# First expert layer of a mixture of experts: 16 products of 128 tokens in place of 8 of 256, per block of hidden units

## The chip, the cores and the metric

The kernel runs on one core of one Trainium2 chip. The metric is the device time of one execution in microseconds; the kernel before has a median of 1494.01 us over two runs (1491.9 and 1496.12).

## What is computed

Three stages follow one another: a recurrent attention, a mixture of eight experts with two experts per token, and a dense two-layer network. The change touches the second, which the reference writes so (N = 3072 tokens, D = 320, E = 8 experts, F = 1024 hidden units):

```python
for e in range(E):
    for k in range(2):
        mask = top2[:, k] == e
        if not mask.any():
            continue
        h = np.maximum(x[mask] @ w1[e], 0.0)
        out[mask] += top2_w[mask, k, None] * (h @ w2[e])
```

## The kernel before

The function `stage_re` first routes: it sorts the (token, expert) pairs by expert into tiles of TS = 256 rows, 31 tiles in all (NTS), each belonging to one expert. The routing ends with small products at line 1000 that turn positions into source rows. Then the function `tile` runs once per tile on every engine; tiles 0, 1 and the last are written out, the others run in a loop of two.

All products of a tile are done in the type float32r, and each operand is split into a high part and a low remainder, so that a product of two operands is three matmuls: high by high, high by low and low by high. ScalarE writes the high parts (`split_hi`, line 814), VectorE the remainders (`split_lo`, line 819).

On TensorE a tile has three parts:

- First layer (lines 963 to 974). For each of NF = 8 blocks `f` of 128 hidden units, the 320 inputs are taken in slices j = 0, 1 (three matmuls each, lines 970 to 972) and a last slice of 64 inputs, whose high and low rows are stacked to 128 (two matmuls, lines 973 and 974). The stationary operand, which is loaded ahead of each matmul, is a 128 x 128 block of the expert's weights (`w1h`, `w1l`); the moving operand is the tile's 256 tokens (`xh`, `xl`). The eight matmuls of a block add up in one PSUM bank (banks 2 to 5 in turn), and the last one raises the semaphore `e_mm1`.
- The turn of the next tile's rows (`turn`, line 954): six transposes against the identity.
- Second layer (lines 985 to 987). For each block `f` and each half `s` of 128 tokens, three matmuls with the tokens' activations as the stationary operand and 320 columns of `w2h` or `w2l` as the moving one.

ScalarE waits for `e_mm1` of a block before it makes `hh` (line 1029), VectorE then makes the remainder `hl` (line 1104), which the second layer needs, and which frees the PSUM bank for block f + 4. POOL gathers the rows of the tile after next once the transposes of a tile are done (line 1072). SP issues the weight loads.

Each of the 31 tiles thus has 8 x 8 = 64 first-layer matmuls: 1984 in all. In the attention stage the products of line 615 (`rows`) are of plain float32, in which one matmul of the code shows as two records in the trace, each with its own load of weights; those of line 1000 are of float32r, with one record each.

Of the kernel before, what the change touches and what calls it, by code (L numbers as in the profile page):

```python
# [821 lines left out]
def stage_re(nc, st, w_in, w_out, w1, w2, xrow, ysort):  # L822
    ctx = ExitStack()
    with ctx:
        def sb(name, shape, dt=F32):
            return ctx.enter_context(nc.sbuf_tensor(name, shape, dt))

        def sem(name):
            return ctx.enter_context(nc.semaphore(name))
# [5 lines left out]
        NF, NS = F1 // 128, TS // 128  # L835
# [5 lines left out]
        w1h, w1l = (sb(n, [128, 3, F1], F32R) for n in ("w1h", "w1l"))  # L841
        w2h, w2l = (sb(n, [128, NF, DM], F32R) for n in ("w2h", "w2l"))
        xs = sb("xs", [128, 2, NS, DM])
        xh = sb("xh", [128, 3, TS], F32R)
        xl = sb("xl", [128, 2, TS], F32R)
# [48 lines left out]
        q = {n: sem(n) for n in names}  # L894
# [5 lines left out]
        def tiles(eng, tile):  # L900
            tile(0, 0, 0, True, False)
            tile(1, 1, 0, True, False)
            with eng.Fori(1, NTS // 2) as n:
                tile(n * 2, 0, n, False, False)
                tile(n * 2 + 1, 1, n, False, False)
            tile(NTS - 1, 0, NTS // 2, False, True)
# [38 lines left out]
        @block.tensor  # L945
        def _(pe):
            mm = nc.tensor.matmul

            def turn(i, p, n):
                pe.wait_ge(gx[p], n * GX + GX)  # L950
                for j, (k0, kr) in enumerate(KE):
                    for s in range(NS):
                        c0 = (j % 2) * TS + s * 128
                        m = nc.tensor.transpose(ps[j // 2][0:kr, c0:c0 + 128], xs[:, p, s, k0:k0 + kr], ident[:, :])  # L954
                m.then_inc(q["e_tr"], 1)

            def tile(i, p, n, first, final):
                if first and p == 0:
                    turn(0, 0, 0)
                pe.wait_ge(q["e_xl"], i * 2 + 2)  # L960
                pe.wait_ge(q["e_w1l"], i * 3 + 3)
                for f in range(NF):
                    fs = slice(f * 128, f * 128 + 128)
                    o = ps[2 + f % 4][:, 0:TS]
                    if f >= 4:
                        pe.wait_ge(q["e_hl"], i * NF + (f - 3))
                    elif not (first and p == 0):
                        pe.wait_ge(q["e_hl"], i * NF - (3 - f))
                    for j in range(2):
                        mm(o, w1h[:, j, fs], xh[:, j, :], start=(j == 0), stop=False)  # L970
                        mm(o, w1h[:, j, fs], xl[:, j, :], start=False, stop=False)  # L971
                        mm(o, w1l[:, j, fs], xh[:, j, :], start=False, stop=False)  # L972
                    mm(o, w1h[:, 2, fs], xh[:, 2, :], start=False, stop=False)
                    mm(o, w1l[:, 2, fs], xh[:, 2, :], start=False, stop=True).then_inc(q["e_mm1"], 1)  # L974
                if not final:
                    turn(i + 1, 1 - p, n + p)
                if not (first and p == 0):
                    pe.wait_ge(q["e_yA"], i)
                    pe.wait_ge(q["e_yV"], i)
                for f in range(NF):  # L980
                    pe.wait_ge(q["e_hl"], i * NF + f + 1)
                    pe.wait_ge(q["e_w2l"], i * NF + f + 1)
                    for s in range(NS):
                        o, sl = ps[6 + s][:, 0:DM], slice(s * 128, s * 128 + 128)
                        mm(o, hh[:, f, sl], w2h[:, f, :], start=(f == 0), stop=False)  # L985
                        mm(o, hh[:, f, sl], w2l[:, f, :], start=False, stop=False)  # L986
                        m = mm(o, hl[:, f, sl], w2h[:, f, :], start=False, stop=(f == NF - 1))  # L987
                m.then_inc(q["e_mm2"], 1)

            pe.wait_ge(q["r_M"], 1)  # L990
            mf = M.rearrange("p e i -> p (e i)")
            mm(ps[5][:, 0:E * NT], one[:, 0:128], mf, start=True, stop=True).then_inc(q["r_PR"], 1)
            mm(ps[4][:, 0:E * NT], triu[:, :], mf, start=True, stop=True).then_inc(q["r_PR"], 1)
            for z, h in enumerate((slice(0, NH0), slice(NH0, NHI))):
                pe.wait_ge(q["r_hi"], z + 1)
                for j in range(2):
                    for i in range(NT):
                        if z == 0 and i % 12 == 0:
                            pe.wait_ge(q["r_lo"], 2 * j + i // 12 + 1)
                        m = mm(ps[3 + 3 * z][:, h], lows[:, j, i, :], highs[:, j, i, h], start=(j + i == 0), stop=(j * i == NT - 1))  # L1000
                m.then_inc(q["r_Q"], 1)
            tiles(pe, tile)

        @block.scalar
# [486 lines left out]
```

## Time and profile before

| what | value |
| --- | --- |
| median of two runs | 1494.01 us |
| profiled execution | 1499.73 us |
| its span, first to last instruction | 1497.9 us |
| TensorE matmul busy | 1297.3 us, 87% of the span |
| weight loads busy | 1180.8 us, 79% |
| VectorE, ScalarE, POOL busy | 925.8, 656.7, 300.8 us |
| mean granted TensorE clock | 0.909 of full speed |

The profiled execution is 5.7 us (0.4%) above the median of the two timed runs, and 1.8 us of it lie outside the span. The stages follow each other: attention to about 560 us, routing to about 623 us, the expert tiles to about 1101 us, the dense network to the end. In the profile PE is TensorE's matmuls and PEld its weight loads, which run beside the matmuls. Where one matmul follows another, the records overlap, because each holds its own latency: how fast the engine goes is read from the distance between starts, not from the duration of one record.

### The profile page before, as it was taken

What the parts mean: (1) busy time and instruction counts of PE and PEld (TensorE: products, weight loads), DVE (VectorE), ACT (ScalarE), POOL (GpSimd) and SP (SyncE); (2) the same over time, 40 slices, a digit from 0 to 9 for tenths busy, and PEclk for the clock granted to TensorE, in tenths of its full rate; (3) what the DMA queues carried; (4) which work ended last, traced back from release to release, by engine and by line L of the source; (5) the groups of instructions that cost most, each with busy time, mean ns of one, the idle gap of its engine ahead of it and who ended that gap; (6) DMA issues with size and microseconds to landing.
All of it is one profiled execution on the core that took longest, in us unless ns stands there. A gap on an engine that the chain in (4) does not pass through costs nothing. (4 is left out here: it accounts for less than half of the span.)

```text
span 1497.9 us, 40886 instructions
## 1 busy us (share of the span) xinstructions
PE 1297.3 (87%) x16814; PEld 1180.8 (79%) x16814; DVE 925.8 (62%) x1605; ACT 656.7 (44%) x1453; POOL 300.8 (20%) x252
## 2 busy tenths in 40 slices
PE   3449877886989783999999999999949999999998
PEld 3337666675867662999999999999947888888887
DVE  5868578484745404678788787888734445454433
ACT  2314443342534231367677676767623332333332
POOL 3406243162612221211111111111023021020000
PEclk9966888787888995699999999999978999999999
DMA  6743453637232311487777878688712011010000
GB/s 164 194 94 122 124 172 109 153 108 191 95 82 92 104 50 48 136 269 225 259 232 237 258 225 263 211 253 245 226 53 71 18 36 44 10 53 18 0 18 18
DMA packets 158556, 197.77 MB, mean 132 GB/s; under 512 B 62581, under 2 KB 117085, under 8 KB 158429
## 3 DMA queue, kind: packets, MB, share of 16 engines
q1 hardware_dynamic: 134428, 149.66, 33.8%
q10 hardware_dynamic: 18721, 28.20, 6.2%
q0 software_dynamic: 5280, 18.03, 4.2%
q8 instruction: 103, 1.69, 0.5%
q14 instruction: 24, 0.20, 0.0%
HBM read 171.53 MB, written 24.31 MB: 131 GB/s over the span
## 5 line engine op out<-in xcount | busy, mean ns | idle before, releaser
L354 DVE TENSOR_TENSOR prod<-Tl,Lt 128x1 f32<-128x1 f32 (+30 forms) x186 | 147.9, 795 | 80.0 <-DMA Lt<-lscr 74.0
L1279 DVE TENSOR_TENSOR gf<-psM,low 128x512 f32<-128x512 f32 x96 | 66.4, 692 | 182.1 <-ACT low L1317 173.7
L1317 ACT ACTIVATE low<-psM 128x512 f32<-128x512 f32 x96 | 57.6, 600 | 245.3 <-PE psM L1375 218.6
L985 PE MATMUL psE<-w2h,hh 128*128 128x320 f32 x496 | 155.7, 314 | 0.0
L987 PE MATMUL psE<-w2h,hl 128*128 128x320 f32 x496 | 153.3, 309 | 0.0
L986 PE MATMUL psE<-w2l,hh 128*128 128x320 f32 x496 | 153.2, 309 | 0.0
L1072 POOL DMA_INDIRECT xs<-xrow,src x62 | 61.0, 984 | 408.9 <-PE psE L954 370.3
L970 PE MATMUL psE<-xh,w1h 128*128 128x256 f32 x496 | 141.0, 284 | 1.9 <-DVE xh L819 1.9
L971 PE MATMUL psE<-xl,w1h 128*128 128x256 f32 x496 | 140.9, 284 | 0.0
L972 PE MATMUL psE<-xh,w1l 128*128 128x256 f32 x496 | 140.9, 284 | 0.0
L819 DVE TENSOR_TENSOR w2l<-w2t,w2h 128x320 fp32r<-128x320 f32 x248 | 122.1, 492 | 16.8 <-ACT w2h L814 16.8
L1354 PE MATMUL psM<-woh,gh 128*128 128x320 f32 x384 | 120.3, 313 | 5.2 <-DVE gl L819 5.0
L1104 DVE SCALAR_TENSOR_TENSOR hl<-psE,hh 128x256 fp32r<-128x256 f32 x248 | 105.2, 424 | 22.6
L1356 PE MATMUL psM<-woh,gl 128*128 128x320 f32 x384 | 118.6, 309 | 0.0
L1355 PE MATMUL psM<-wol,gh 128*128 128x320 f32 x384 | 118.5, 309 | 0.0
L814 ACT ACTIVATE w2h<-w2t 128x320 fp32r<-128x320 f32 x248 | 115.0, 464 | 5.7 <-DMA w2t<-in_w_dram 5.1
L1029 ACT ACTIVATE hh<-psE 128x256 fp32r<-128x256 f32 x248 | 95.4, 385 | 47.2 <-PE psE L974 46.0
L819 DVE TENSOR_TENSOR w1l<-w1t,w1h 128x1024 fp32r<-128x1024 f32 (+1 forms) x93 | 108.1, 1218 | 2.0
L814 ACT ACTIVATE w1h<-w1t 128x1024 fp32r<-128x1024 f32 x93 | 91.4, 1050 | 13.9 <-DMA w1t<-in_w_dram 13.9
L970 PEld LDWEIGHTS psE<-xh,w1h 128*128 128x128 f32 x496 | 95.6, 193 | 2.3 <-DVE xh L819 2.3
L358 DVE TENSOR_REDUCE Tl<-prod 128x1 f32<-128x1 f32 (+30 forms) x186 | 93.7, 504 | 5.9
L972 PEld LDWEIGHTS psE<-xh,w1l 128*128 128x128 f32 x496 | 95.8, 193 | 0.0
(182 smaller groups left out, 3140.0 us busy)
## 6 DMA issues: line engine op xcount, KB each, us to landing
w2t<-in_w_dram SPq DMA_DIRECT2D x31, 1280.0 KB, 6.8
w1t<-in_w_dram SPq DMA_DIRECT2D x31, 1024.0 KB, 8.7
w1t<-in_w_dram SPq DMA_DIRECT2D x62, 256.0 KB, 9.3
Vd<-in_vG_dram ACTq DMA_DIRECT2D x44, 320.0 KB, 5.0
ysort<-ys SPq DMA_DIRECT2D x31, 320.0 KB, 4.9
RV<-in_rvE_dram ACTq DMA_DIRECT2D x44, 208.0 KB
P<-in_wR_dram SPq DMA_DIRECT2D x24, 209.6 KB
U<-in_wE_dram SPq DMA_DIRECT2D x24, 209.6 KB
```

The costliest lines, as they stand in the source:

```text
L354: mark(nc.vector.tensor_tensor(prod[:, 0:t, 0:t], Tl[:, 0:t, CH - t:CH], Lt[:, t:t + 1, CH - t:CH].to_broadcast([128, t, t]), ALU.mult))
L814: return nc.scalar.activation(hi, src, ACT.Copy)
L819: return nc.vector.tensor_tensor(lo, src, hi.bitcast(F32), ALU.subtract)
L970: mm(o, w1h[:, j, fs], xh[:, j, :], start=(j == 0), stop=False)
L971: mm(o, w1h[:, j, fs], xl[:, j, :], start=False, stop=False)
L972: mm(o, w1l[:, j, fs], xh[:, j, :], start=False, stop=False)
L985: mm(o, hh[:, f, sl], w2h[:, f, :], start=(f == 0), stop=False)
L986: mm(o, hh[:, f, sl], w2l[:, f, :], start=False, stop=False)
L987: m = mm(o, hl[:, f, sl], w2h[:, f, :], start=False, stop=(f == NF - 1))
L1354: mm(o, gh[:, f % 4, sl], woh[:, f, :], start=(f == 0), stop=False)
L1355: mm(o, gh[:, f % 4, sl], wol[:, f, :], start=False, stop=False)
L1356: m = mm(o, gl[:, f % 4, sl], woh[:, f, :], start=False, stop=(f == NF - 1))
```

## The change

The eight matmuls of a block are issued twice, first for tokens 0 to 127 and then for tokens 128 to 255 (NS = 2), each with 128 moving columns and into its own half of the same PSUM bank. Every matmul of the second half loads the weights anew that its partner in the first half had loaded. The semaphore is raised once, by the sixteenth matmul.

```diff
-                    for j in range(2):
-                        mm(o, w1h[:, j, fs], xh[:, j, :], start=(j == 0), stop=False)
-                        mm(o, w1h[:, j, fs], xl[:, j, :], start=False, stop=False)
-                        mm(o, w1l[:, j, fs], xh[:, j, :], start=False, stop=False)
-                    mm(o, w1h[:, 2, fs], xh[:, 2, :], start=False, stop=False)
-                    mm(o, w1l[:, 2, fs], xh[:, 2, :], start=False, stop=True).then_inc(q["e_mm1"], 1)
+                    for z in range(NS):
+                        zs = slice(z * 128, z * 128 + 128)
+                        oz = o[:, zs]
+                        for j in range(2):
+                            mm(oz, w1h[:, j, fs], xh[:, j, zs], start=(j == 0), stop=False)
+                            mm(oz, w1h[:, j, fs], xl[:, j, zs], start=False, stop=False)
+                            mm(oz, w1l[:, j, fs], xh[:, j, zs], start=False, stop=False)
+                        mm(oz, w1h[:, 2, fs], xh[:, 2, zs], start=False, stop=False)
+                        m = mm(oz, w1l[:, 2, fs], xh[:, 2, zs], start=False, stop=True)
+                    m.then_inc(q["e_mm1"], 1)
```

On TensorE, at the start of a tile inside the loop, the block that goes to bank 2 (psE2) and the first matmul of the next block (psE3) stand so before the change; behind the names are the columns of the weights and of the moving operand:

```order
L970 MATMUL psE2<-xh,w1h 128x256 [waits e_hl,e_w1l,e_xl]
L971 MATMUL psE2<-xl,w1h 128x256
L972 MATMUL psE2<-xh,w1l 128x256
L970 MATMUL psE2<-xh,w1h 128x256
L971 MATMUL psE2<-xl,w1h 128x256
L972 MATMUL psE2<-xh,w1l 128x256
L973 MATMUL psE2<-xh,w1h 128x256
L974 MATMUL psE2<-xh,w1l 128x256
L970 MATMUL psE3<-xh,w1h 128x256 [waits e_hl]
```

The last rows of the same block in the changed program, on the same engine, from the second half's first matmul on (lines 973 to 977 are the old 970 to 974):

```order
L973 MATMUL psE2<-xh,w1h 128x128
L974 MATMUL psE2<-xl,w1h 128x128
L975 MATMUL psE2<-xh,w1l 128x128
L973 MATMUL psE2<-xh,w1h 128x128
L974 MATMUL psE2<-xl,w1h 128x128
L975 MATMUL psE2<-xh,w1l 128x128
L976 MATMUL psE2<-xh,w1h 128x128
L977 MATMUL psE2<-xh,w1l 128x128
L973 MATMUL psE3<-xh,w1h 128x128 [waits e_hl]
```

The eight rows of one block have become sixteen, of half the moving columns and with the same waits ahead of the first; nothing else on TensorE, and nothing on any other engine, has moved.

## Rows read from the trace of the kernel before

**Rows 1.** Page: busy time of TensorE; its clock in 40 slices.
```profile
PE 1297.3 (87%) x16814; PEld 1180.8 (79%) x16814; DVE 925.8 (62%) x1605; ACT 656.7 (44%) x1453; POOL 300.8 (20%) x252
PEclk9966888787888995699999999999978999999999
```
**Rows 2.** Windows: length, then busy PE, PEld, DVE, ACT, POOL; clock, DMA share, GB/s.
```profile
600.00:1100.00 500.00, 497.74 (x3744) 497.16 (x3745) 393.59 (x738) 326.29 (x714) 61.03 (x62) 0.97 0.73 228
```
**Rows 3.** Groups by line: busy us, mean ns of one, idle before (us).
```profile
L970 PE MATMUL psE<-xh,w1h 128*128 128x256 f32 x496 | 141.0, 284 | 1.9 <-DVE xh L819 1.9
L971 PE MATMUL psE<-xl,w1h 128*128 128x256 f32 x496 | 140.9, 284 | 0.0
L972 PE MATMUL psE<-xh,w1l 128*128 128x256 f32 x496 | 140.9, 284 | 0.0
L973 PE MATMUL psE<-xh,w1h 128*128 128x256 f32 x248 | 70.3, 284 | 0.0
L974 PE MATMUL psE<-xh,w1l 128*128 128x256 f32 x248 | 70.3, 283 | 0.0
```
**Rows 4.** Timeline of PE over one tile: start us, us, then the instruction.
```profile
855.93 0.28 PE L970 MATMUL psE<-xh,w1h 128*128 128x256 f32 x1
...
863.61 0.82 PE L954 MATMUL psE<-ident,xs 128*128 128x128 f32 x6
864.18 0.39 PE L985 MATMUL psE<-w2h,hh 128*128 128x320 f32 x1
...
871.30 0.28 PE L970 MATMUL psE<-xh,w1h 128*128 128x256 f32 x1
```
**Rows 5.** Timeline of the weight loads of line 1000.
```profile
599.37 10.32 PEld L1000 LDWEIGHTS psE<-woh,wih 128*128 128x128 f32 x48 [9.74 <-issue]
610.17 10.31 PEld L1000 LDWEIGHTS psE<-woh,wih 128*128 128x128 f32 x48 [0.49 <-DVE woh L1180]
```
**Rows 6.** Groups by line, line 1000 and the loads of the first layer.
```profile
L1000 PE MATMUL psE<-woh,wih 128*128 128x56 f32 x48 | 10.4, 394 | 0.4 <-DVE woh L1180 0.4
L1000 PE MATMUL psE<-woh,wih 128*128 128x6 f32 x48 | 10.4, 353 | 9.3 <-DVE wih L1186 9.3
...
L1000 PEld LDWEIGHTS psE<-woh,wih 128*128 128x128 f32 x96 | 20.6, 332 | 10.2 <-issue 9.7 <-DVE woh L1180 0.5
...
L972 PEld LDWEIGHTS psE<-xh,w1l 128*128 128x128 f32 x496 | 95.8, 193 | 0.0
```
**Rows 7.** Timeline: the products of line 615, at full and at half clock.
```profile
211.40 1.86 PEld L615 LDWEIGHTS psA<-wx,xT 104*128 104x128 f32 x16 [0.19 <-issue]
211.40 2.02 PE L615 MATMUL psA<-wx,xT 104*128 104x96 f32 x16
...
566.96 3.49 PEld L615 LDWEIGHTS psA<-wx,xT 104*128 104x128 f32 x16 [0.95 <-DVE xT L378]
```
**Rows 8.** Windows: the granted clock is the third number from the right.
```profile
599.40:620.40 21.00, 20.60 (x96) 20.51 (x96) 14.66 (x11) 3.13 (x4) 5.05 (x4) 0.50 0.29 66
623.83:627.04 3.21, 3.21 (x15) 3.21 (x16) 0.00 (x0) 0.00 (x0) 0.62 (x1) 0.50 1.07 397
627.04:1101.00 473.96, 473.96 (x3638) 473.96 (x3638) 378.20 (x724) 322.30 (x708) 54.08 (x56) 1.00 0.75 234
128.00:132.00 4.00, 3.34 (x157) 2.89 (x156) 2.29 (x6) 1.35 (x4) 3.78 (x3) 1.00 0.02 4
132.00:136.00 4.00, 3.57 (x135) 2.61 (x138) 3.90 (x4) 1.03 (x1) 4.00 (x2) 0.51 0.26 67
```
**Rows 9.** Waits: engine, line, releaser: us in total, times, longest us.
```profile
POOL xs L1072 <- PE psE L954: 364.3, 28, 13.2
...
ACT hh L1029 <- PE psE L974: 46.0, 214, 0.2
```
**Rows 10.** Timeline of PE in the first tile.
```profile
623.83 0.58 PE L970 MATMUL psE<-xh,w1h 128*128 128x256 f32 x1 [1.86 <-DVE xh L819]
...
633.01 0.82 PE L954 MATMUL psE<-ident,xs 128*128 128x128 f32 x6
```

## The prediction

> **What bounds the kernel now.** I began with the page: TensorE's matmuls fill 87% of the span, more than any other engine's work, and its clock is high through the middle [rows 1]. The windows by stage say where that counts: in the 500 us of the expert tiles the matmuls are busy 497.7 us, VectorE 394 and ScalarE 326 [rows 2]. The groups of the first layer show idle time ahead of one line only, 1.9 us in all [rows 3]. From the first tile to the last, matmuls and loads leave no gap (the long window in [rows 8]). The waits confirm it from the other side: ScalarE waits 214 times for the last matmul of a block, and POOL 28 times for the transposes [rows 9]. So in this stage TensorE waits for nobody and everyone waits for it. Whatever is added to its time lengthens the kernel one for one; whatever the others gain is worth nothing.
>
> The timeline of one tile gives the rates. The first layer lasts from 855.93 to 863.61, 7.68 us for 64 matmuls: one each 120 ns. The transposes take 0.57 us, the second layer 7.12 us, and the tile 15.37 us [rows 4]. At full clock (2.4 GHz) 256 columns stream in 106.7 ns, so each matmul costs about 13 ns beyond its columns. Over 31 tiles the first layer has 1984 matmuls (3 x 496 + 2 x 248 in [rows 3]).
>
> **The change part by part.** It removes 1984 matmuls of 256 columns and adds 3968 of 128. The columns streamed stay the same; the weight loads double. If a matmul's distance to the next were set by its columns alone, 128 columns would cost 53.3 + 13.3 = 66.7 ns, a pair 133 instead of 120, and the sum would be 1984 x 13.3 ns = +26 us. The question is whether a load of 128 weight columns fits into 67 ns. Now it need fit only into 120.
>
> The rows of line 1000 answer it best: the same type, the same 128 x 128 weights, and only 6 and 56 moving columns. The 48 loads of either kind take 10.3 us [rows 5]; less the duration of the last load, 0.33 us [rows 6], this is 9.98 / 47 = 212 ns from start to start, for 6 columns as for 56. The clock there is 0.50, that is 1.2 GHz (the first window in [rows 8]), so columns would account for 5 and 47 ns. The distance is 256 periods of that clock whatever the columns are: the load is the limit, at two periods for each of its 128 columns. In the durations the moving columns do count singly: 394 - 353 = 41 ns for 50 more columns [rows 6], 0.83 ns each, one period at 1.2 GHz. At full clock the load's 256 periods are 106.7 ns.
>
> Line 615 shows the same limit at both clocks. These are float32 records, each with 128 weight columns and 96 moving ones. At half clock the loads follow each other every (3.49 - 0.33) / 15 = 211 ns; at full clock every (1.86 - 0.19) / 15 = 111 ns [rows 7], where 0.33 and 0.19 us are one load's duration at either clock [rows 6]. The matmul row of the same group, with a last record of about 0.28 us, gives (2.02 - 0.28) / 15 = 116 ns [rows 7]. I take 112 ns per matmul, since the group of 16 holds its start-up and the new train of 128 has few starts. The lower bound is 106.7 ns, the load at full clock with nothing around it. The upper is 120 ns, which the present matmuls reach with that load beside them [rows 4].
>
> By the Trainium skill, page "TensorE: Matmul & The Clock Gate", section "LDWEIGHTS (loading the stationary operand)", a load takes its weight columns over 1.2 GHz, 107 ns, and no other clock is named for it. By that the sum would be 1984 x (214 - 120) = +186 us. The trace agrees at full clock (111) and not at half (212).
>
> Sum. In 30 tiles a first layer goes from 64 x 120 to 128 x 112 ns, 7.68 to 14.34 us: +6.66 us, in all +199.7 us. Bounds: 93 to 120 ns for each of 1920 pairs, +179 to +230 us.
>
> The first tile starts at half clock. With 256 columns the clock rose after 3.2 us (the second and third window in [rows 8]), and its first layer took 633.01 - 623.83 = 9.18 us [rows 10]. In the 20.6 us of line 1000, with loads back to back and short matmuls between them, it did not rise (the first window in [rows 8]). The changed stream is like the second of these, with the load as its limit, so I take that it stays low through the first tile's first layer: 128 x 213 ns = 27.3 us, +18.1 us; then the second layer starts low, some 12 matmuls of 320 columns at 267 instead of 147 ns, +1.4 us. Together +19.5. If it rises after 3.2 us as before: 15 matmuls at 213 and 113 at 112 are 15.9 us, +6.7. These are the ends.
>
> What else moves costs nothing. The semaphore `e_mm1` still comes once a block, 1.79 us apart instead of 0.96. ScalarE and VectorE have their `hh` and `hl` done sooner relative to TensorE, so the waits for `e_hl` stay hidden. If that cover were gone, each block would cost one pass of both; nothing here makes them later. The gathers and weight loads have 6.7 us more per tile. The second layer, the transposes and the other stages stay.
>
> Total +199.7 + 19.5 = +219 us. The profiled execution becomes 1499.7 + 219 = 1719 us; the median of the runs shown is 5.7 us lower, so I predict 1713 us. The ends are 1494 + 179 + 7 = 1680 and 1494 + 230 + 20 = 1744.
>
> **The rivals.**
> 1. The load is no floor at full clock, and only the columns count: +26 us, 1520 us, 1.8% more and so not told from no change, since a measurement of this kernel tells about 2%. It holds if a load fits into 67 ns at full clock; it is worth nothing from 107 ns on. For it: loads and matmuls do overlap, and 1000's rows are at half clock. Against it: 111 ns at full clock on line 615, and 193 ns recorded for one load of the first layer at full clock against 332 at half [rows 6], a ratio of a scaled load plus a fixed part. Between this and my value, the Trainium skill, same page, section "Back-to-back issue gap", gives about 81 ns for each pair of load and matmul of 128 columns: 1984 x (162 - 120) = +83 us, 1577 us. No row of this kernel shows 128 weight columns loaded that fast.
> 2. The array does narrow float32r products at a lower rate, four passes over the columns in place of one: 213.3 + 13.3 = 227 ns for 128 columns, a pair 453, and 1984 x 333 = +661 us, 2155 us. For it: four passes of at least 64 columns would also give the 213 ns of line 1000. Against: 41 ns for 50 columns is one pass, and these products have one record each, where float32 has two. Two passes would be hidden under the load, and change nothing.
> 3. The clock falls in the first layers, which become a stream of loads with short matmuls. It did fall elsewhere while PE was busy 3.34 of 4 us with small matmuls (the last two windows in [rows 8]). If all first layers ran at half: 1984 x (427 - 120) = +609 us, 2103 us; with half of them, about 1800 to 1910. Against: the small matmuls there have at most 40 weight columns or 40 rows and gaps between them; here the whole array is used with no gap, and each tile has 7 us of dense second layer.
>
> **How the numbers follow.** My forecast, load-limited at full clock, 0.82; rival 1 0.05 (two fifths of it near 1520, the rest near 1577); rival 2 0.07; rival 3 0.06. The range 1676 to 1755 is that of the forecast's bounds with the scatter of a few us, and leaves out the rivals, 0.18. Slower by over 2% is everything but the stream-limited case: 0.97; within 2% 0.02; faster by over 2% 0.01, for what I do not see.
>
> **What would show each step.** Right: in the tiles' timeline, starts of the first-layer matmuls 107 to 120 ns apart, 14.3 us from the first to the transposes, 22.0 us per tile; the clock 1.00 from the second tile on; the second layer still 7.1 us; no new idle on TensorE. The first tile's first layer of 27 us shows its clock. Wrong: a distance of 67 to 81 ns (rival 1), of 227 with the clock at 1.00 (rival 2), or of 213 with the clock at 0.50 (rival 3).

## The result

The changed kernel has a median of 1713.74 us over two runs (1712.55 to 1714.94), against 1494.01 us before: a ratio of 1.1465, with a 95% interval from 1.1419 to 1.1512. It is 15% slower. The prediction was 1713, with a range of 1676 to 1755.

The page of the profiled execution (span 1713.1 us), its busy times, its clock, and the two largest groups of the first layer with one of its loads:

```profile
PE 1513.4 (88%) x18798; PEld 1396.7 (82%) x18798; DVE 932.4 (54%) x1605; ACT 655.9 (38%) x1453; POOL 302.9 (18%) x252
...
PEclk9968888878889558999999999999999799999999
...
L975 PE MATMUL psE<-xh,w1l 128*128 128x128 f32 x992 | 278.0, 280 | 0.0
L974 PE MATMUL psE<-xl,w1h 128*128 128x128 f32 x992 | 277.8, 280 | 0.0
...
L973 PEld LDWEIGHTS psE<-xh,w1h 128*128 128x128 f32 x992 | 194.8, 196 | 2.3 <-DVE xh L819 2.3
```

Against [rows 1], TensorE has 216 us more, in 1984 more records, and the other engines as many instructions as before. Against [rows 3], 992 matmuls of 128 columns stand where 496 of 256 stood, and one of them lasts 280 ns, as long as one of twice the columns did (284). The first experiment shows why: with the same 128 moving columns a record lasts 222 ns beside 32 or 64 weight columns and 276 beside 128, so it holds a wait for the weights.

The timeline: the start and the end of the first tile's first layer, then one later tile, as in [rows 4]:

```profile
623.09 0.47 PE L973 MATMUL psE<-xh,w1h 128*128 128x128 f32 x1 [1.86 <-DVE xh L819]
...
650.45 1.50 PE L954 MATMUL psE<-ident,xs 128*128 128x128 f32 x6
651.61 0.61 PE L989 MATMUL psE<-w2h,hh 128*128 128x320 f32 x1
...
872.17 0.84 PE L954 MATMUL psE<-ident,xs 128*128 128x128 f32 x6
872.77 0.39 PE L989 MATMUL psE<-w2h,hh 128*128 128x320 f32 x1
...
879.88 0.22 PE L973 MATMUL psE<-xh,w1h 128*128 128x128 f32 x1
...
893.90 0.28 PE L976 MATMUL psE<-xh,w1h 128*128 128x128 f32 x1
894.01 0.28 PE L977 MATMUL psE<-xh,w1l 128*128 128x128 f32 x1
```

The next transposes start at 894.12, so a first layer takes 14.24 us for 128 matmuls, 111.3 ns each, and the tile 894.12 - 872.17 = 21.95 us instead of 15.37. From the transposes to the first matmul of the next tile it is 7.71 us, where [rows 4] had 7.69: in the later tiles nothing else has moved, and their whole loss is in the distance of the first layer's starts.

The windows: the first tile's first layer, then to the rise of the clock, then all later tiles (granted clock third from the right, as in [rows 8]).

```profile
623.09:650.45 27.36, 27.36 (x128) 27.36 (x129) 6.32 (x15) 5.55 (x15) 0.60 (x1) 0.50 0.34 110
650.45:655.17 4.72, 4.72 (x20) 4.65 (x21) 2.81 (x5) 3.50 (x6) 2.15 (x2) 0.50 1.01 355
655.17:1320.77 665.60, 663.32 (x5490) 663.06 (x5489) 371.78 (x706) 313.43 (x689) 51.78 (x55) 1.00 0.52 162
```

The first tile ran at half clock throughout its first layer, 27.36 us against 9.18 in [rows 10]. The clock rose 4.7 us after that: the six transposes took 1.16 us of it (650.45 to 651.61) where they take 0.60 in the later tile (872.17 to 872.77), and the second layer's first 3.6 us ran at half clock too. Then the clock stayed up. The waits of the later tiles, as in [rows 9]:

```profile
ACT hh L1033 <- PE psE L977: 244.4, 240, 1.0
DVE hl L1108 <- ACT hh L1033: 218.6, 240, 0.9
```

ScalarE now waits 1 us for every block, five times as long in all, and VectorE behind it. These waits cost nothing: the tile got longer only by what TensorE's own distances explain.

### The profile page after: what moved, and what is told of

It reads as the page before. It is cut to its first block and busy times, and to the rows that moved or that the text cites. A ratio compares the mean times of both kernels' runs of the same rounds, so it can differ in the third digit from the quotient of the medians.

```text
span 1713.1 us, 44854 instructions
## 1 busy us (share of the span) xinstructions
PE 1513.4 (88%) x18798; PEld 1396.7 (82%) x18798; DVE 932.4 (54%) x1605; ACT 655.9 (38%) x1453; POOL 302.9 (18%) x252
## 5 line engine op out<-in xcount | busy, mean ns | idle before, releaser
L975 PE MATMUL psE<-xh,w1l 128*128 128x128 f32 x992 | 278.0, 280 | 0.0
L974 PE MATMUL psE<-xl,w1h 128*128 128x128 f32 x992 | 277.8, 280 | 0.0
L973 PE MATMUL psE<-xh,w1h 128*128 128x128 f32 x992 | 275.2, 277 | 1.9 <-DVE xh L819 1.9
L973 PEld LDWEIGHTS psE<-xh,w1h 128*128 128x128 f32 x992 | 194.8, 196 | 2.3 <-DVE xh L819 2.3
L975 PEld LDWEIGHTS psE<-xh,w1l 128*128 128x128 f32 x992 | 195.0, 197 | 0.0
L974 PEld LDWEIGHTS psE<-xl,w1h 128*128 128x128 f32 x992 | 194.9, 196 | 0.0
L354 DVE TENSOR_TENSOR prod<-Tl,Lt 128x1 f32<-128x1 f32 (+30 forms) x186 | 152.0, 817 | 76.7 <-DMA Lt<-lscr 70.6
L976 PE MATMUL psE<-xh,w1h 128*128 128x128 f32 x496 | 139.6, 282 | 0.0
L977 PE MATMUL psE<-xh,w1l 128*128 128x128 f32 x496 | 137.6, 277 | 0.0
```

The source lines that it names most:

```text
L354: mark(nc.vector.tensor_tensor(prod[:, 0:t, 0:t], Tl[:, 0:t, CH - t:CH], Lt[:, t:t + 1, CH - t:CH].to_broadcast([128, t, t]), ALU.mult))
L973: mm(oz, w1h[:, j, fs], xh[:, j, zs], start=(j == 0), stop=False)
L974: mm(oz, w1h[:, j, fs], xl[:, j, zs], start=False, stop=False)
L975: mm(oz, w1l[:, j, fs], xh[:, j, zs], start=False, stop=False)
L976: mm(oz, w1h[:, 2, fs], xh[:, 2, zs], start=False, stop=False)
```

## The experiments

The question is what sets 111 ns for a matmul of 128 columns, when 256 columns cost 120. The theory: the load of 128 four-byte weight columns, two clock periods for each column. The rivals: a lower rate for narrow products (two passes over the columns give nearly the same 107 + 13 = 120 ns, so the result alone can't tell them apart); a cost per matmul that has nothing to do with the weights' size or type; and, beside these, the clock.

**One shape for each block.** One kernel whose eight blocks differ in weight columns and in the cut of the tokens:

```diff
+HALVES = (slice(0, 128), slice(128, 256))
+CURVE = ((128, HALVES), (96, HALVES), (64, HALVES), (32, HALVES), (128, (slice(0, 256),)), (96, (slice(0, 256),)), (128, (slice(0, 224), slice(224, 256))), (128, (slice(0, 64), slice(64, 256))))
...
-                    for z in range(NS):
-                        zs = slice(z * 128, z * 128 + 128)
-                        oz = o[:, zs]
+                    wc, parts = CURVE[0 if first and p == 0 else f]
+                    fs = slice(f * 128, f * 128 + wc)
+                    for zs in parts:
+                        oz = o[0:wc, zs]
```

> The changed kernel, but from the second tile on each of the eight blocks of the first layer has a shape of its own: weight columns x moving columns are 128x128, 96x128, 64x128, 32x128, 128x256, 96x256, then 128 weight columns with the tokens cut 224+32, then 64+192. Blocks with fewer than 128 weight columns leave the other hidden units out of the computation. Theory (a load of 128 four-byte weight columns is the floor, two clock periods per weight column plus 5 ns, 111.7 ns in all; columns plus 13.3 ns otherwise): distances of 112, 85, 67 and 67 ns in the first four blocks, 120 and 120 in the next two, and 112 for every matmul of the last two, whatever its columns; a first layer of about 10.8 us, the whole about 1608 us. Rival (narrow float32r matmuls take two passes over their columns): 120 ns in each of the first four blocks whatever the weights, 200 and 40 ns in the 224+32 block, 67 and 173 ns in the 64+192 block (if 192 counts as narrow; 93 if not).

The kernel leaves out part of the hidden units, and its time, 1597.0 us in one run, is read as that of the instruction stream. The timeline of one tile, the first matmul of some of its parts:

```profile
709.87 0.28 PE L977 MATMUL psE<-xl,w1h 128*128 128x128 f32 x1
...
711.54 0.25 PE L976 MATMUL psE<-xh,w1h 128*96 128x128 f32 x1
...
712.91 0.23 PE L976 MATMUL psE<-xh,w1h 128*64 128x128 f32 x1
...
713.87 0.22 PE L976 MATMUL psE<-xh,w1h 128*32 128x128 f32 x1
...
714.83 0.33 PE L976 MATMUL psE<-xh,w1h 128*128 128x256 f32 x1
...
717.64 0.19 PE L976 MATMUL psE<-xh,w1h 128*128 128x32 f32 x1
...
718.46 0.28 PE L976 MATMUL psE<-xh,w1h 128*128 128x64 f32 x1
...
719.35 0.34 PE L976 MATMUL psE<-xh,w1h 128*128 128x192 f32 x1
```

The first number after the operands' names is rows by weight columns, the second holds the moving columns. Fifteen matmuls of 128 weight columns take 711.54 - 709.87 = 1.67 us, 111 ns each; sixteen of 96 take 1.37 us, 86 ns; sixteen of 64, and sixteen of 32, take 0.96 us, 60 ns; eight of 64 tokens take 0.89 us, 111 ns. The medians of the distances over all tiles:

| weight columns | moving columns | ns, start to start |
| --- | --- | --- |
| 128 | 32 | 112 |
| 128 | 64 | 112 |
| 128 | 128 | 111 |
| 128 | 192 | 111 |
| 128 | 224 | 113 |
| 128 | 256 | 119 |
| 96 | 128 | 86 |
| 96 | 256 | 117 |
| 64 | 128 | 60 |
| 32 | 128 | 60 |

Down a column of moving widths from 32 to 224 nothing changes: the load alone counts. Down the weight columns at 128 tokens the distance falls by 25 ns for 32 columns, 0.8 ns a column, which is two periods at 2.4 GHz (0.83), until at 64 the 128 moving columns take over at 60 ns. Two passes would have left 120 ns in these four rows. Where the distance no longer shows the load, its own record does. The loads of line 978 from 660 to 1200 us, at full clock, by weight columns:

```profile
L978 PEld LDWEIGHTS psE<-xh,w1l 128*128 128x128 f32 x416 | 79.6, 191 | 0.0
...
L978 PEld LDWEIGHTS psE<-xh,w1l 128*96 128x96 f32 x176 | 28.7, 163 | 0.0
...
L978 PEld LDWEIGHTS psE<-xh,w1l 128*64 128x64 f32 x116 | 15.6, 135 | 0.0
...
L978 PEld LDWEIGHTS psE<-xh,w1l 128*32 128x32 f32 x117 | 12.7, 109 | 0.0
```

From 128 to 32 weight columns one load's mean record falls from 191 to 109 ns, 0.85 ns a column: again two periods each. The theory stands. One number of mine does not: 128 columns with a load that fits beside them cost 53 + 7 = 60 ns, not the 53 + 13 = 67 that I had carried over from the 256-column matmuls. The whole was 11 us below the expected 1608, most of it from this: 7 ns x 32 matmuls x 30 tiles are 7 us.

**An uneven cut.** The same number of matmuls, 192 + 64 tokens:

```diff
-                    for z in range(NS):
-                        zs = slice(z * 128, z * 128 + 128)
+                    for zs in (slice(0, 192), slice(192, 256)):
```

> The changed kernel with the tokens cut 192+64 in place of 128+128. Theory (load floor of 111.7 ns per matmul): no difference from the changed kernel, 1714 us, and again a first tile at half clock. Rival (two passes for matmuls under 256 columns): 173 ns for 192 columns and 67 to 112 for 64, a pair 240 to 285 in place of 223, 1984 x 17 to 62 ns more: 1747 to 1837 us. If columns alone counted: the same 133 ns per pair as for 128+128.

Measured: 1712.0 us, ratio 1.1461 (1.1409 to 1.1512), a tile of 21.96 us, the first tile's first layer again at half clock. That is within 0.01 us of the changed kernel's tile. The cost goes by the number of loads, not by the width of what follows them. The clock of all later tiles, third number from the right:

```profile
648.18:1313.78 665.60, 663.61 (x5492) 663.34 (x5491) 372.76 (x707) 314.30 (x690) 52.44 (x55) 1.00 0.52 162
```

It holds at 1.00, with 64-column matmuls in every block. Two later experiments come back to this.

**The first tile whole.**

```diff
-                    for z in range(NS):
-                        zs = slice(z * 128, z * 128 + 128)
+                    for zs in ((slice(0, TS),) if first and p == 0 else (slice(0, 128), slice(128, 256))):
```

> The changed kernel, but the first tile keeps its 64 matmuls of 256 tokens. My term for the first tile (half clock all through its first layer, then a slow start of the second layer) says that its first layer falls from 27.4 to 9.2 us, with the clock up after some 3 us, and that the whole loses 18 to 20 us: about 1694 us. Rival: the clock stays low there for another reason (what ran before the tile) and rises when it did in the changed kernel: then the first tile's 64 matmuls take 13.7 us at 213 ns, and the whole is 1700 us or more.

Measured: 1689.3 us, ratio 1.1306 (1.1268 to 1.1343). Its timeline, and the window up to the rise of the clock:

```profile
615.28 0.58 PE L972 MATMUL psE<-xh,w1h 128*128 128x256 f32 x1 [1.86 <-DVE xh L819]
...
625.15 0.82 PE L954 MATMUL psE<-ident,xs 128*128 128x128 f32 x6
```

```profile
600.00:620.08 20.08, 17.82 (x82) 17.24 (x83) 7.87 (x13) 2.54 (x8) 6.96 (x6) 0.50 0.45 147
```

The first layer of this tile takes 9.87 us instead of 27.36, and the next tile has its transposes 21.94 us later instead of 24.12: 19.7 us regained in the trace. The clock rose at 620.08, 4.8 us into the first layer, where in the changed kernel it stayed down for 27 us on the same work in narrower pieces. So the term for the first tile was real and is caused by the cut itself, not by what ran before. The median is 24.4 us below the changed kernel's, more than the 19.7; the rest is within the scatter of the stages ahead, for this execution reached the expert layer at 615.28 us and the changed kernel's at 623.09.

**A quarter of the matmuls cut.** Only the last slice of 64 inputs, lines 973 and 974 of the kernel before:

```diff
-                    mm(o, w1h[:, 2, fs], xh[:, 2, :], start=False, stop=False)
-                    mm(o, w1l[:, 2, fs], xh[:, 2, :], start=False, stop=True).then_inc(q["e_mm1"], 1)
+                    for zs in (slice(0, 128), slice(128, 256)):
+                        mm(o[:, zs], w1h[:, 2, fs], xh[:, 2, zs], start=False, stop=False)
+                        m = mm(o[:, zs], w1l[:, 2, fs], xh[:, 2, zs], start=False, stop=(zs.stop == TS))
+                    m.then_inc(q["e_mm1"], 1)
```

> Only the last slice of 64 inputs, two of the eight matmuls of a block, is cut into 128+128 tokens: 496 of the 1984 matmuls become 992. Theory: a block goes from 8 x 120 to 6 x 120 + 4 x 111.7 = 1167 ns, +207 ns x 248 = +51 us, 1545 us, plus up to 6 us if the first tile stays at half clock. If columns alone counted: +7 us. Two passes: +60 us. So a split costs by the number of matmuls cut, a quarter of the whole change's steady part.

Measured: 1535.2 us, ratio 1.0303 (1.0249 to 1.0358), that is +37 to +53 us. The tile is 16.95 us, +1.58 against +1.66 expected; 30 tiles make +47 us, and the first tile, whose clock rose in its first layer, +2. A quarter of the cuts costs a quarter of the 6.58 us a tile (1.65), within 5%: the cost goes in proportion to the matmuls cut, as far as these two points show.

**The same weights twice in a row.** If the array kept its weights, the second half could go without a load. Two twins with 15 matmuls a block, the shared weights next to each other or seven matmuls apart. The new lines of the first twin; its twin has the loop over the halves outermost:

```diff
+                    both = (slice(0, 128), slice(128, 256))
+                    mm(o, w1h[:, 0, fs], xh[:, 0, :], start=True, stop=False)
+                    for j in range(3):
+                        for a, b in ((w1h, xh), (w1h, xl), (w1l, xh)):
+                            if (j == 0 and a is w1h and b is xh) or (j == 2 and b is xl):
+                                continue
+                            for zs in both:
+                                m = mm(o[:, zs], a[:, j, fs], b[:, j, zs], start=False, stop=(j == 2 and a is w1l and zs.stop == TS))
```

> The changed kernel with the two matmuls that share their weights issued one right after the other (halves innermost); the first product of a block stays whole, so a block is 1 + 14 matmuls. Theory (each matmul pays for its own load, even of the weights that are already in the array): 120 + 14 x 112 = 1684 ns a block, a first layer of 13.5 us, a tile of 21.1 us; 1494 + 30 x 5.8 + 15 = about 1683 us. Rival (a second matmul with the same weights skips or shortens its load): pairs of 112 + 60 ns, a block of 1324 ns, first layer 10.6 us, about 1597 us.

> The twin of the kernel with adjacent pairs: the same 1 + 14 matmuls a block, but all seven of the first half, then all seven of the second, so that no two neighbours share their weights. Theory: the same time as its twin, 1683 us. Rival: slower than the twin by up to 7 x 52 ns a block, 86 us.

Measured: 1677.2 us adjacent (ratio 1.1199, 1.1167 to 1.1232) and 1684.4 apart (1.1247, 1.1214 to 1.1281). The intervals overlap, and the tile is 21.12 us in both; the profiled execution of the second had reached the expert stage 9.1 us later (first transposes at 620.2 and 611.1 us), in code that the twins share. The timeline of the adjacent kernel shows the pairs as one row each:

```profile
677.05 0.39 PE L976 MATMUL psE<-xh,w1l 128*128 128x128 f32 x2
677.27 0.39 PE L976 MATMUL psE<-xh,w1h 128*128 128x128 f32 x2
677.50 0.39 PE L976 MATMUL psE<-xl,w1h 128*128 128x128 f32 x2
```

A pair with the same weights takes 0.22 us, two full loads: in both twins every first-layer matmul of the code has a load of its own in the trace, 3720 of each. Nothing is saved by order.

**Two-byte operands.** All first-layer matmuls on constant bfloat16 tiles:

```diff
-                        for j in range(2):
-                            mm(oz, w1h[:, j, fs], xh[:, j, zs], start=(j == 0), stop=False)
...
+                        for k in range(8):
+                            m = mm(oz, wb[:, :], xb[:, zs], start=(k == 0), stop=(k == 7))
```

> The changed kernel's 128 first-layer matmuls a tile, of 128 weight and 128 moving columns, but on constant two-byte (bfloat16) operands: the first layer's real products are left out. Theory (the floor is the reading of four-byte weights at two clock periods a column): with two-byte weights the load takes at most half, 53 ns, and the columns set the distance, about 60 ns; a first layer of 7.7 us, a tile of 15.3 us, a whole near 1494 us. Rival (the floor is a fixed cost of 128 weight columns of any type): 112 ns and 1714 us again.

Measured: 1475.1 us in one run. One first layer in the timeline, and the transposes behind it; then the group of its loads at full clock:

```profile
635.01 7.32 PE L974 MATMUL psE<-xb,wb 128*128 128x128 bf16 x128
642.17 0.82 PE L955 MATMUL psE<-ident,xs 128*128 128x128 f32 x6
```

```profile
L974 PEld LDWEIGHTS psE<-xb,wb 128*128 128x128 bf16 x3751 | 209.5, 98 | 3.0
```

128 matmuls take 7.16 us, 56 ns each, where the four-byte ones take 111. With two-byte operands the load is hidden behind 128 columns (53.3 ns at 2.4 GHz), and a cost for 128 weight columns of any type is excluded. The load is still there in the trace, and its record lasts 98 ns. By the loads of the first experiment, half the bytes would be like 64 four-byte columns, 135 ns, and even 32 of those take 109; so the number of bytes alone does not explain it. Not separated here: both operands changed their type, and one constant block served all loads. An uncut two-byte kernel was not run, so what the cut would cost there is not shown. The operands are constants, and the first layer is not computed; the time is read as that of the instruction stream.

**Three parts.** The cut taken further, 128 + 64 + 64:

```diff
-                    for z in range(NS):
-                        zs = slice(z * 128, z * 128 + 128)
+                    for zs in (slice(0, 128), slice(128, 192), slice(192, 256)):
```

> The changed kernel with the tokens cut 128+64+64: 24 matmuls a block instead of 16. Theory: the load floor again per matmul, 192 x 111.7 = 21.4 us a first layer, 29.1 us a tile, and the first tile at half clock: 192 x 213 = 41 us; in all 1494 + 30 x 13.8 + 33 = about 1940 us, and the clock stays at 1.00 in all later tiles. Rival on the clock: with even fewer columns between the loads it falls to 0.50 in the first layers, up to 192 x 213 = 41 us each, 2100 to 2500 us.

Measured: 2440.7 us, ratio 1.6298 (1.6251 to 1.6345). The rival on the clock had it. The windows of one cycle and of the next stretch at full clock, cut where the clock changes:

```profile
657.01:667.25 10.24, 10.24 (x82) 10.24 (x81) 5.78 (x10) 3.69 (x8) 1.56 (x1) 1.00 0.58 153
667.25:704.80 37.55, 37.55 (x174) 37.48 (x174) 8.77 (x17) 8.55 (x18) 1.89 (x2) 0.50 0.24 74
704.80:715.03 10.23, 10.23 (x84) 10.23 (x83) 3.20 (x6) 1.59 (x5) 0.00 (x0) 1.00 0.34 92
```

TensorE is never idle, 174 loads and matmuls in 37.55 us, and yet it runs at 1.2 GHz. The clock rises in the second layer of each tile, by turns 2.8 and 4.4 us after it has begun, stays up for 10.24 us, and falls again in the first layer of the next one; it is down for 37.55 and 34.13 us by turns, and a tile takes 46.1 us. The load is the floor at both levels: for 64 as for 128 moving columns the median distance is 111 to 112 ns at full clock, 213 at half.

**Between the two.** Even blocks in two parts, odd blocks in three:

```diff
-                    for z in range(NS):
-                        zs = slice(z * 128, z * 128 + 128)
+                    for zs in ((slice(0, 128), slice(128, 256)) if f % 2 == 0 else (slice(0, 128), slice(128, 192), slice(192, 256))):
```

> Between the changed kernel and the one of three parts: even blocks cut 128+128, odd blocks 128+64+64, 160 matmuls in a first layer. If the clock holds at 1.00 as in the changed kernel: 160 x 111.7 = 17.9 us a first layer, 25.5 us a tile, and 160 x 213 = 34.1 us in the first tile; about 1494 + 30 x 10.2 + 26 = 1826 us. If it falls as with three parts, a tile lies between 25.5 and 41 us: 2000 to 2300 us. The three-part run shows that a fall is possible, not where it begins; I give the fall 0.5.

Measured: 2218.1 us, ratio 1.4841 (1.4734 to 1.4948), a tile of 39.3 us. The clock falls here as well:

```profile
654.08:664.32 10.24, 10.24 (x81) 10.24 (x81) 6.00 (x10) 3.92 (x8) 1.79 (x1) 1.00 0.59 164
664.32:695.03 30.71, 30.71 (x143) 30.64 (x143) 8.55 (x17) 8.55 (x18) 1.89 (x2) 0.50 0.28 91
```

With the clock up it would have been about 1826. The changed kernel, with 128 loads a tile, loses 6.6 us a tile and keeps its clock at 1.00; this one, with 160, loses 23.9, where 10 would have come from the loads alone. The 64-column matmuls are not enough to explain the fall: the uneven cut has them too, with 128 loads, and held 1.00 for 665.60 us. What in the stream the fall hangs on is not shown.

**The finding turned to use.** In line 1000 the load is 128 columns wide and the moving operand 6 or 56. Exchanging them makes the load small:

```diff
-                        m = mm(ps[3 + 3 * z][:, h], lows[:, j, i, :], highs[:, j, i, h], start=(j + i == 0), stop=(j * i == NT - 1))
+                        m = mm(ps[3 + 3 * z][0:n, 0:128], highs[:, j, i, h], lows[:, j, i, :], start=(j + i == 0), stop=(j * i == NT - 1))
...
```

The result, now 6 or 56 rows by 128, is copied once and transposed back.

> The kernel before, with the roles of the operands exchanged at line 1000: the 6 or 56 position columns become the weights and the 128 rows the moving operand, and each of the two small results is turned back by one copy and one transpose. If the load of 128 columns was what held these 96 matmuls at 213 ns at half clock, they now go at the rate of their 128 moving columns, 107 to 112 ns: the second 48 take 5.3 instead of 10.4 us, less about 0.5 us for the copy and the transpose. The first 48 gain little, as VectorE makes their operands until about 604 us. The second group ends the wait for the first tile, so the whole gains 4 to 5 us: 1489 against 1494, 0.3%. Rival (a fixed cost per float32r matmul at half clock): 213 ns again, and about 1 us slower.

> The kernel with exchanged roles at line 1000 once more, since its gain of the first measurement (0.9974, from 0.9946 to 1.0003) was as large as its interval. Its own trace has 3.8 us less from the first of these matmuls to the first one of the expert layer, 0.25%: so 0.9975 again if that is all. Rival (the trace's gain is taken back behind it): 1.000.

The timeline of the first measurement:

```profile
594.74 3.02 PE L1006 MATMUL psE<-wih,woh 128*6 128x128 f32 x24 [9.26 <-DVE wih L1197]
...
605.51 1.53 PE L1006 MATMUL psE<-wih,woh 128*56 128x128 f32 x12 [4.97 <-DVE woh L1191]
...
607.17 3.54 PE L1006 MATMUL psE<-wih,woh 128*56 128x128 f32 x36
...
615.40 0.58 PE L971 MATMUL psE<-xh,w1h 128*128 128x256 f32 x1 [1.86 <-DVE xh L819]
```

The median distance of these 96 matmuls is 107 ns at half clock, where [rows 5] had 212, and 60 at full clock. TensorE now waits 4.97 us for VectorE's operands. From the first of these matmuls to the expert layer it is 615.40 - 594.74 = 20.66 us instead of 623.83 - 599.40 = 24.43: 3.8 us less, and 3.2 less in the trace of the second measurement. But the times were 0.9974 (0.9946 to 1.0003) and then 0.9993 (0.9959 to 1.0027) of before: no difference that this measurement can tell. The load theory is borne out once more, at the other level of the clock; as an improvement of the kernel it is not shown.

## Why the prediction was right

- *TensorE sets the time of this stage, one for one.* Right. 30 tiles x 6.58 us and the terms of the first tile make 218 us; the span grew by 215.2.
- *The load of 128 weight columns takes the place of the columns as the limit, taken at 112 ns.* Right: 111.3 ns over a first layer. The reading from line 1000 at half clock and line 615 at full clock was the deciding step, and the experiments showed its mechanism: independent of the moving columns from 32 to 224, proportional to the weight columns from 128 to 96, gone with two-byte weights. The steady term was +199.7 and came to 197.4.
- *The first tile stays at half clock, +18.1, and its second layer starts low, +1.4.* Right in its cause, a little low in size. The first part was 27.36 - 9.18 = 18.2 us. The second was 24.12 - 21.95 = 2.2 us, counted from the transposes of the first tile to those of the next. My 1.4 left out the six transposes between the layers, which ran at half clock as well: 1.16 us where a later tile has 0.60, so 0.6 us more. The second layer itself had 3.6 us at half clock, 13 matmuls where I had counted 12, so 1.6 us more.
- *Nothing else moves.* Right for the later tiles: 7.71 against 7.69 us for the rest of a tile. In the first tile the transposes moved, as just said.
- *Rival 1, columns alone.* Wrong in its condition, for a load of 128 weight columns takes 111 ns at full clock and not 67; and its price was too high, for by the 60 ns of the first experiment the pair would have cost 120 ns and not 133, that is nothing at all. The intermediate case, the 81 ns of the Trainium skill's page "TensorE: Matmul & The Clock Gate", section "Back-to-back issue gap", is not what any product of 128 weight columns took here: the four-byte ones are above it, at 111 ns, and the two-byte ones below it, at 56.
- *Rival 2, several passes.* Wrong: 60 ns for 128 moving columns beside 64 weight columns is one pass. One remark on it was wrong too: two passes would not have changed nothing. At 120 ns for 128 columns they would have exceeded the load's 112 and given the upper bound of my sum; the first experiment, not the result, excluded them clearly.
- *Rival 3, the clock.* It did not happen in the change, but I held it to be less likely than it deserved. I argued that the small matmuls near which the clock had fallen used only a part of the array and had gaps between them. The kernels with 160 and 192 loads a tile use the whole array, have no gap, and fall all the same, the first of them to 2218.1 us. The change, at 128 loads, may stand close to a loss of 700 us, and the 0.06 was an argument that happened to hold. The price was short as well: it counted the first layers alone, and with three parts the clock stayed down through the transposes and up to 4.4 us of the second layer.

The agreement to 1 us is partly luck: the stages ahead of the experts, which are the same code in most of these kernels, differ by up to 12 us between executions (the first transposes of the expert stage start at 608.7 us in one trace and at 620.4 in another), and the ends of my sum were 64 us apart.

## What to carry to other kernels

A matmul of this code pays for its own load of weights, even of those that are there already (21.12 us a tile with equal weights adjacent or apart). With four-byte weights the load costs two clock periods a weight column (0.85 ns at 2.4 GHz), why two is not shown, so each matmul should stream about twice as many columns as its weights have: 128 weight columns took 111 to 113 ns with 32 to 224 moving columns and 119 with 256. Below that the time goes by the number of matmuls and the columns come for nothing. Where one operand is narrow, let the narrow one be the weights: at half clock that brought line 1000 from 212 to 107 ns a matmul. And look at the granted clock of every variant: the streams of 160 and 192 loads a tile ran at 1.2 GHz for most of the time, with TensorE busy all along.

## What was not expected

- The clock falls in a stream without a gap: with three parts to half for 34 or 38 us of each 46.1 us tile, with TensorE busy all along; and it does so already with 160 loads a tile, where it did not with 128. Between the two nothing was tried.
- What a matmul costs beyond its columns is not constant. At full clock it is 13 ns with 256 columns and a load of 128 weight columns (119 to 120 ns), 10 ns with a load of 96 (117), and 7 ns with 128 columns beside a load of 64 or 32 (60 ns); with two-byte operands 2.6 ns (55.9).
- The cut has a cost at the start of the stage that is large for one tile: in 27 us of the 128 four-byte matmuls of 128 columns the clock did not come up, where with the 64 of 256 columns it came after 3.2 to 4.8 us. The width of the matmul alone is not the reason: the two-byte kernel has 128 matmuls of 128 columns in its first tile, and its clock came up after 4.06 us. Its two windows of that first layer:

```profile
618.24:622.30 4.06, 4.06 (x39) 4.06 (x40) 0.04 (x1) 0.54 (x2) 0.60 (x1) 0.50 1.06 398
622.30:627.31 5.01, 5.01 (x92) 5.01 (x91) 5.01 (x14) 4.63 (x14) 0.00 (x0) 1.00 0.83 257
```
